# Writing out the loops of a three-stage attention and mixture kernel, dropping three fillers, and reordering its end

## The reference

```python
# attention: phi(x)[i*8+j] = (S1 x)[i] * (S2 x)[j]
kv = einsum('bhsf,bhsd->bhfd', phi(k), v);  z = phi(k).sum over s
x = (phi(q) @ kv) / (phi(q) @ z + 1e-6)            # N = 4352 tokens, D = 128
# first mixture: (token, expert) pairs by falling logit, capacity 544 each
out[mask_e] = relu(x[mask_e] @ w1[e]) @ w2[e]      # F = 1024
# second mixture: 32 slots
logits = x @ phi
d = softmax(logits, over tokens);  slot_input = d.T @ x
slot_out[e] = relu(slot_input[e] @ u1[e]) @ u2[e]
c = softmax(logits, over slots);   return c @ slot_out
```

## Time and profile before

| | us |
|---|---|
| median of 3 runs | 378.01 |
| lowest, highest | 373.85, 380.95 |
| profiled execution | 379.05 |
| its span, first to last instruction | 377.3 |

### The profile page before, as it was taken

The page is one execution under the profiler, slowest core; times in us unless marked ns, Lnnn a source line. Parts: engine busy times, 40 slices in busy tenths (PEclk is TensorE's granted clock), DMA queues, the critical chain, the costliest instruction groups (busy, mean ns, idle before and its releaser), DMA issues.

```text
span 377.3 us, 7253 instructions
## 1 busy us (share of the span) xinstructions
PE 314.6 (83%) x2583; PEld 237.4 (63%) x2592; DVE 209.7 (56%) x859; ACT 91.6 (24%) x189; POOL 86.3 (23%) x104
## 2 busy tenths in 40 slices
PE   7999999623344997888989899898898998998963
PEld 4699999612233674666657667566676786754552
DVE  3535479977888675576557647756683100303253
ACT  1331234200000221321411231231142344412332
POOL 4000100000014022505323151350526163403100
PEclk9999999955555798999869779898989999999987
DMA  7999204120021020202202202110311313000106
GB/s 248 405 413 422 117 2 113 56 69 3 20 93 31 0 64 25 63 9 76 61 2 69 71 7 56 37 55 0 85 57 30 116 23 130 7 2 5 63 2 237
DMA packets 15029, 31.58 MB, mean 84 GB/s; under 512 B 2848, under 2 KB 8864, under 8 KB 13984
## 3 DMA queue, kind: packets, MB, share of 16 engines
q1 hardware_dynamic: 11584, 27.46, 21.1%
q0 software_dynamic: 2560, 2.79, 2.9%
q10 hardware_dynamic: 864, 1.05, 0.8%
HBM read 26.28 MB, written 5.01 MB: 83 GB/s over the span
## 4 chain that ended last, share of the span: by engine, by line
PE 65%; DVE 14%; issue 5%; DMA 5%; POOL 4%; another core or an unknown queue 2%; ACT 2%; SPq 0%; ACTq 0%; POOLq 0%; DVEq 0%
PE psum L523 15%; PE psum L531 15%; PE psum L418 5%; PE psum L617 5%; PE psum L431 4%; DVE feats L1129 3%; PE psum L402 3%; PE psum L550 2%; POOL kq_sb L370 2%; PE psum L563 2%; POOL slot_logits_by_token L380 2%; PE psum L627 1%; DMA slot_logits_by_token<-kq_sb,tokens 1%; PE psum L642 1%
## 5 line engine op out<-in xcount | busy, mean ns | idle before, releaser
L531 PE MATMUL psum<-v_flat,kq_sb 128*128 128x272 f32 x256 | 83.5, 440 | 0.4 <-ACT v_flat L834 0.4
L523 PE MATMUL psum<-kq_sb 128*128 128x272 f32 x256 | 81.0, 434 | 0.8 <-ACT kq_sb L827 0.8
L370 POOL DMA_INDIRECT kq_sb<-x_by_token,tokens x40 | 41.5, 1037 | 129.6 <-DVE tokens L1108 117.9
L834 ACT ACTIVATE v_flat<-psum 128x544 f32<-128x544 f32 x64 | 39.9, 624 | 114.9 <-PE psum L523 92.2
L380 POOL DMA_INDIRECT slot_logits_by_token<-kq_sb,tokens x40 | 39.1, 978 | 81.0 <-ACT kq_sb L863 71.2
L523 PEld LDWEIGHTS psum<-kq_sb 128*128 128x128 f32 x256 | 47.6, 203 | 11.2 <-issue 1.6
L531 PEld LDWEIGHTS psum<-v_flat,kq_sb 128*128 128x128 f32 x256 | 46.7, 201 | 9.2 <-ACT v_flat L834 1.7
L1129 DVE TENSOR_TENSOR feats<-digit_pad,steps 128x640 bf16<-128x640 int16 (+1 forms) x86 | 43.3, 537 | 0.3
L617 PE MATMUL psum<-mask_pad,feats 128*128 128x32 bf16 (+1 forms) x490 | 22.4, 180 | 22.1 <-DVE feats L1129 18.6
L617 PEld LDWEIGHTS psum<-mask_pad,feats 128*128 128x128 bf16 x490 | 19.1, 100 | 30.5 <-DVE feats L1129 13.7
L1205 DVE CAST partial<-psum 128x32 f16<-128x32 f32 (+1 forms) x42 | 7.8, 185 | 38.2 <-PE psum L617 29.2
(11 more groups left out here) (230 smaller groups left out, 436.2 us busy)
## 6 DMA issues: line engine op xcount, KB each, us to landing
u_sb<-u SPq DMA_DIRECT2D x8, 1024.0 KB, 19.4
kq_sb<-wts SPq DMA_DIRECT2D x16, 512.0 KB, 3.6
kq_sb<-kT SPq DMA_DIRECT2D x4, 512.0 KB, 5.7
v_flat<-v SPq DMA_DIRECT2D x4, 512.0 KB, 6.6
kq_sb<-qT SPq DMA_DIRECT2D x4, 512.0 KB, 8.5
x_by_token<-x SPq DMA_DIRECT2D x4, 512.0 KB, 3.2
out<-x SPq DMA_DIRECT2D x4, 256.0 KB, 3.4
out<-x ACTq DMA_DIRECT2D x3, 256.0 KB, 3.6
```

What stands on the lines that cost most here:

```text
L370: pool.indirect_dma_start(out=xg[0:rows, b, :], out_offset=None, in_=x_dram, in_offset=bass.IndirectOffsetOnAxis(ap=tokens[0:rows, which, ...
L523: mm = pe.matmul(psum[:, 2 + 2 * (f % 2) + half, 0:HALF], w_sb[:, f // HALF_CHUNKS, f % HALF_CHUNKS], xsT[:, half * HALF:(half + 1) * HALF ...
L531: mm = pe.matmul(psum[:, 6 + half, 0:HALF], w_sb[:, f // HALF_CHUNKS, HALF_CHUNKS + f % HALF_CHUNKS], hT[:, f % 2, half * HALF:(half + 1) ...
L834: act.activation(hT[:, f % 2].rearrange("p (b t) -> p b t", b=2), psum[:, 2 + 2 * (f % 2):4 + 2 * (f % 2), 0:HALF], ACT.Relu)\
```

## The change

Four things are done. The `Fori` loops of SP, POOL, PE, ACT and DVE over phases 2 to 6 become Python loops, so that the code of the five passes is written out, with constants for all waits. The two `keep_warm` calls of the hand-over (three fillers) are removed from these phases. ACT's exponential of the slot-side softmax is moved behind all four copies to `h2T`, and is cut, as DVE's maximum, subtraction and sum are, into two groups (five and four of the nine groups of tiles). And the normalisation is moved: PE transposes the exponentials as they are, and the reciprocal is applied when the output is copied out of PSUM, by a multiply on DVE and by the scale operand on ACT, there tile by tile. For uniform groups the logits are padded to 36 tiles by a small memset on POOL.

```diff
-            with pe.Fori(2, PHASES) as i:
+            for i in range(2, PHASES):
                 phase(i, True, True)
...
                 if network:
                     pe.wait_ge(S["y_copied"], i - 1)
-                    keep_warm(7, 2)
                     outputs(i - 2)
-                    keep_warm(7, 1)
...
-            pe.wait_ge(S["c_ready"], 1)
             for n, quads in enumerate(QUAD_BANKS):
                 for j, g in enumerate(quads):
+                    if g in (0, QUADS_A):
+                        pe.wait_ge(S["rexp_ready"], 1 if g == 0 else 2)
-                    mm = pe.transpose(psum[0:len(CG[g]) * SLOTS, 3 + n, j * P:(j + 1) * P],
-                                      c_quads[:, g, 0:len(CG[g]), :].rearrange("p q s -> p (q s)"), ident[:])
+                    mm = pe.transpose(psum[:, 3 + n, j * P:(j + 1) * P],
+                                      c_quads[:, g].rearrange("p q s -> p (q s)"), ident[:])
                 mm.then_inc(S["c_turned"], 1)
...
             for n in range(4):
-                if n == 2:
-                    act.wait_ge(S["rshift_ready"], 1)
-                    act.activation(l2t, l2t, ACT.Exp).then_inc(S["rexp_ready"], 1)
                 act.wait_ge(S["h2t_ready"], n + 1)
                 act.copy(h2T[...], psum[...]).then_inc(S["h2t_copied"], 1)
+            for n, (a, z) in enumerate(((0, QUADS_A), (QUADS_A, PER_QUAD))):
+                act.wait_ge(S["rshift_ready"], n + 1)
+                act.activation(c_quads[:, a:z], c_quads[:, a:z], ACT.Exp).then_inc(S["rexp_ready"], 1)
...
+            act.wait_ge(S["c_ready"], 1)
             for n in range(1, len(OUT_BANKS), 2):
                 act.wait_ge(S["out_ready"], n + 1)
-                act.copy(o_sb[:, tiles[0]:tiles[-1] + 1], psum[...]).then_inc(S["out_copied_a"], 1)
+                for i, t in enumerate(tiles):
+                    ins = act.activation(o_sb[:, t], psum[:, 4 * (w % 2) + q, i * P:(i + 1) * P], ACT.Copy,
+                                         scale=rr[:, t - PER_QUAD * q, q:q + 1])
+                ins.then_inc(S["out_copied_a"], 1)
...
             dve.wait_ge(S["l2_loaded"], 16)
-            step(dve.tensor_reduce(rmax[:], l2t, AX.X, ALU.max))
-            dve.tensor_tensor(l2t, l2t, rmax[...], ALU.subtract).then_inc(S["rshift_ready"], 1)
-            dve.wait_ge(S["rexp_ready"], 1)
-            step(dve.tensor_reduce(rs[:], l2t, AX.X, ALU.add))
+            for a, z in quad_groups:
+                step(dve.tensor_reduce(rmax[:, a:z], l2_quads[:, a:z], AX.X, ALU.max))
+                dve.tensor_tensor(c_quads[:, a:z], l2_quads[:, a:z], rmax[...], ALU.subtract)\
+                    .then_inc(S["rshift_ready"], 1)
+            for n, (a, z) in enumerate(quad_groups):
+                dve.wait_ge(S["rexp_ready"], n + 1)
+                step(dve.tensor_reduce(rs[:, a:z], c_quads[:, a:z], AX.X, ALU.add))
             step(dve.tensor_scalar(rs[:], rs[:], 1e-9, None, ALU.add))
-            step(dve.reciprocal(rr[:], rs[:]))
-            dve.tensor_tensor(c_quads[:, :, 0:3, :], l2t[...], rr[...], ALU.mult)
-            dve.tensor_tensor(c_quads[:, 0:FULL_QUADS, 3, :], l2t[...], rr[...], ALU.mult).then_inc(S["c_ready"], 1)
+            dve.reciprocal(rr[:], rs[:]).then_inc(S["c_ready"], 1)
...
             for n in range(0, len(OUT_BANKS), 2):
-                dve.tensor_copy(o_sb[...], psum[...]).then_inc(S["out_copied_v"], 1)
+                dve.tensor_tensor(o_sb[...], psum[...], rr[...], ALU.mult).then_inc(S["out_copied_v"], 1)
```

More of the change, by code:

```diff
@@ L46 @@
 PER_QUAD = -(-TILES // 4)
-FULL_QUADS = TILES - 3 * PER_QUAD
+QUADS_A = 5
 YW = D + 1
@@ L195, in build @@
         so8 = sb("so8", [P, P], F32)
[L196 to L198 removed]
+        rmax = sb("rmax", [P, PER_QUAD, 4], F32)
+        rs = sb("rs", [P, PER_QUAD, 4], F32)
+        rr = sb("rr", [P, PER_QUAD, 4], F32)
         def parts(flat, total, *sizes):
@@ L255, in build @@
         abg = [(w, g) for w in range(2) for g in range(NG)]
-        CG = [list(range(g, TILES, PER_QUAD)) for g in range(PER_QUAD)]
-        QUAD_BANKS = [list(range(g, min(g + 4, FULL_QUADS))) for g in range(0, FULL_QUADS, 4)] + \
-            [list(range(FULL_QUADS, PER_QUAD))]
+        QUAD_BANKS = [list(range(g, min(g + 4, PER_QUAD))) for g in range(0, PER_QUAD, 4)]
         rows_of = [P] * (BLOCKS - 1) + [TAIL]
@@ L301, in load_expert @@
                 for h in range(2):
-                    if not isinstance(turn, int) or turn:
+                    if turn:
                         sp.wait_ge(S["chunk_done"], CHUNKS * turn - CHUNKS + HALF_CHUNKS * (h + 1))
@@ L307, in _ @@
             load_expert(0, 0, 1)
-            with sp.Fori(2, PHASES) as i:
+            for i in range(2, PHASES):
                 load_expert(i - 1, 0, i)
@@ L387, in _ @@
             gather(0, 1)
-            with pool.Fori(2, PHASES) as i:
+            for i in range(2, PHASES):
                 gather(i - 1, 1)
@@ L873, in _ @@
             copy_rows(0)
-            with act.Fori(2, PHASES) as i:
+            for i in range(2, PHASES):
                 network(i - 2)
@@ L928, in step @@
                 ins.then_inc(S["dve_step"], 1)
-                dve.wait_ge(S["dve_step"], base[0] + count[0])
+                dve.wait_ge(S["dve_step"], count[0])
             def features(n):
@@ L1297, in _ @@
             phase(1, True, False)
-            so_far = count[0]
-            with dve.Fori(2, PHASES) as i:
-                count[0] = 0
-                base[0] = PER_PHASE * (i - 2) + so_far
+            for i in range(2, PHASES):
                 phase(i, True, True)
-                assert count[0] == PER_PHASE, count[0]
-            base[0] = PER_PHASE * (PHASES - 2) + so_far
-            count[0] = 0
-            after(0)
+            after(count[0])
             dve.tensor_scalar(turn_id[:, 1:2], fwsum[:], -1.0, float(EXPERTS), ALU.mult, ALU.add)\
```

44 lines of the change are left out of this document (17 added, 27 removed).

## The result

| | before, us | after, us | ratio, 95% interval |
|---|---|---|---|
| median (4 runs each) | 376.75 | 362.72 | 0.963 [0.956, 0.969] |
| profiled execution | 379.05 | 363.32 | |
| its span | 377.3 | 361.6 | |

The changed kernel is 14.0 us faster by the medians, 15.7 in the profiled pair.

The account below looks back on a forecast made before the run. PE's own work was taken to bound the kernel (65% of the chain). From 379.05 us, 0 for loops, 3.2 for fillers and 2.5 for the end left 373.35, less 1.04 for the median: 372.3 us, range 363.5 to 378.0.

Parts of the forecast that it names:

- Part 1, the loops: Phases 2 to 6 written out as straight code on all engines: costed at 0, since PE's back edge costs nothing measurable.
- nameless waits go with the loop: Looped phases: straight code removes DVE's 8.5 us of unexplained waits at its copy of partial sums, 363.8 us; chance 0.16.
- Part 2, the fillers: Three fillers less in each of five hand-overs, 0.21 us each on PE: 3.2 us saved, between zero and 6.4.
- Part 3, the end: Second softmax and output: output matmuls 4.2 us earlier, output copies 1.7 us later, net gain 2.5 us.
- the last one: Output copies at the end: ACT's scaled copies take longer, so the end comes 1.7 us later (0.3 to 3.2).
- The clock: Phases 2 to 6 without fillers: mean clock falls by 0.055, 379.3 us, chance 0.12; by 0.11, 386.3 us, chance 0.04.
- price of 0.4 us lost for each us at 1.2 GHz: Phases 3 and 4, same code: the clock alone explains most of their 3.77 us difference, about 0.4 us per half-level us.
- Fetching straight code: Written-out passes: code run for the first time stalls on fetching in four more passes, +5.2, so 377.5 us; chance 0.10.

Follow-up runs that it names:

- rebalanced end: Changed kernel with loops put back and one four-tile output bank moved from ACT to DVE: 370.72 us, against 369.01 of the same kernel without the move.

## Why the prediction was wrong, point by point

**Part 1, the loops: the step that failed.** "I cost this part at 0." At the 347 level that is right (1.004 and 0.9995). At the level at which the prediction's own trace was taken, the loops cost 8.9 to 9.7 us. I had looked for their cost at the back edge and found none, which holds: the hand-over lost one filler and nothing else. The cost lies elsewhere in the pass, at level 5, where PE's result reaches DVE after some 1.6 us instead of 0.85: 0.7 us in each of phases 3 to 6, 2.8 us. The trace of the kernel before showed this wait, and I did not ask what it would be without the loop. The remaining 6 to 7 us go with time at 1.2 GHz, of which looped kernels had more, and with a first pass that is 2.5 us longer in two of four. That PE's idle time brings the lower clock about is argued from the two coming together, not shown by an experiment of its own.

The stall is not one of fetching. DMA queues of the kernel before from 150 to 276 us (packets, MB, share of 16 engines), and of the changed kernel from 146 to 265:

```profile
DMA packets 2432, 5.59 MB, mean 44 GB/s; under 512 B 832, under 2 KB 1152, under 8 KB 2432
## 3 DMA queue, kind: packets, MB, share of 16 engines
q1 hardware_dynamic: 1152, 4.19, 11.5%
q0 software_dynamic: 1280, 1.40, 4.5%
```

```profile
q8 instruction: 7, 0.11, 0.4%
q14 instruction: 5, 0.04, 0.1%
```

The loops fetch nothing in these four passes (phases 3 to 6), the written-out code twelve packets, and at the 347 level the loops cost nothing. The Trainium skill ("Runtime: NRT & Kernel Launch", on instruction fetch mechanics) says that a taken branch out of the fetched blocks stalls on a fetch; it had the right sign here, but by these rows not the mechanism.

**The rival "nameless waits go with the loop"** gave 363.8 us, which is near the result for a reason that does not hold. The waits stayed (8.5 and 8.9 us). They are the visible part of a larger lateness, in which most waits carry PE's name and so looked like ordinary waits: 29.2 us at DVE's copy of the partial sums before, 21.4 after, 13.1 at the 347 level; with the nameless ones 37.7, 30.3 and 13.1. I judged the mechanism by four waits without a name, where the sum of all waits at this line was to be compared.

**Part 2, the fillers.** 0.21 us each was to give 0.64 us a phase; at equal clock it is 0.43 to 0.46 us at the 347 level and 0.49 at 377 (28.36 with the fillers put back, 27.87 without), so 2.2 to 2.5 us of the 3.2. Why they cost less than their length is open. Of this only 0.6 to 0.9 us arrive in the time of the kernel at 347 when nothing else is changed, but 2.3 when the loops are written out too (345.52 against 347.81). At 377 it is 3.7 us, not separable from 2.5. No new wait took their place.

**Part 3, the end.** Right in mechanism: 6.35 us to the first output matmul (6.7 forecast), ACT's four-tile bank 1.14 us (1.2), the second half of slot outputs 1.95 us without waiting. The gain is 3.4 to 3.5 us alone by the medians, and 4.3 in the profiled pair (from the landing of the logits to the end of the span, 20.4 to 16.1), against 2.5. The term that was mis-sized is the last one: from the first output matmul to the end of the span 9.75 us, not 11.2. ACT's last copy ends 1.9 us later than before, counted from there (7.51 us against 5.64; 1.7 forecast), but the tail behind it shrank from 3.8 to 2.2 us. I had kept the tail fixed; by the rates of the rebalanced end it is the landing of the queue of output transfers, and there 1.6 us less on ACT gave only 0.4.

**The clock** was to fall, if anything, without the fillers. It rose: 0.88 to 0.94 in the mean over phases 3 to 6, with the loops gone. What the fillers alone do to it is not settled. The profiled execution with them put back has less time at 1.2 GHz, 8.5 us against 12.9 and 15.2 without them, which is the way the rival had it; the means of four whole executions each are the same, 0.903 and 0.905. The price of 0.4 us lost for each us at 1.2 GHz, read from phases 3 and 4, was too high: phase 4 also holds a late result at level 2 (DVE waits 1.91 us there, 0.26 in phase 3), and the means of the table above give 0.3 (4.1 us for 14.0). **Fetching straight code** stalls nothing: 20 packets instead of 13, and at the 347 level phases 4 to 6 take 25.0 us either way.

## What to carry to other kernels

A wait that no record explains, and waits with an ordinary name that are longer in one phase than in its twin, can be one thing: sum up all waits at the line, and compare instruction by instruction with a stretch or a run in which nothing is late, before a part of the change is costed at nothing. A loop should be priced over the whole pass, not at its back edge. And take the price of an engine's indirect transfers from a run without them: here they cost the kernel some 4 to 5% of its time at one of its two levels, for the most part through another engine. (An estimate: 0.963 or 0.9575 times 371.5 is 356 to 358 us, less 339.45, of which 2 to 3 us also came without late results.)

## What the runs showed of the hardware

- The same kernel runs at 347 us or at 371 to 377 us, in sets on chips with the same number too; nearly all of the difference is in phases 2 to 6 (phases 3 to 6 of kernels with fillers mostly 25.0 us, against 28.0 to 32.7), while the stages ahead of them (117 to 121 us) and the second turn behind (18.6 to 19.1 us) are alike. What decides between the levels was not found.
- At the 377 level PE's results come up to 2 us late to DVE around the indirect DMAs that POOL issues, 3.3 us a phase at full clock; with plain DMAs of the same bytes they do not, and at the 347 level neither do they with the indirect ones. By which path POOL's issuing reaches PE's results is open.
- At that level hardware loops on all five engines cost 0.7 us more in each of phases 3 to 6 (a wait of 1.53 to 1.66 us instead of 0.75 to 0.90, 16 phases each) and come with a lower clock (24 against 10 us at 1.2 GHz in the mean of four profiled executions each); at the 347 level they cost nothing. On which engine the loop matters is open.
- One ACT activation of 128 columns out of PSUM with a per-partition scale takes 0.37 us, 0.10 more than a plain copy (0.27); four in a row take 1.14 us, 0.29 each.
